# Attention and two MoE blocks on one core: q and k given head dimension first, scores from stacked high and low parts

## What is computed

```python
scores = scale * np.matmul(q, k.transpose(0, 1, 3, 2))      # scale = 1/8
rel = pos[:, None] - pos[None, :]
bias = slopes[:, None, None] * (-np.abs(rel).astype(np.float32))[None, :, :]
mask = (rel >= 0) & (rel < 128)
scores = np.where(mask, scores + bias[None], -1000000000.0)
attn = exp(scores - max) / (sum + 1e-09)
x = (attn @ v) as (2304 tokens, 512)
x = relu(x @ w_in) ** 2 @ w_out                             # w_in 512 x 2048
logits = x @ w_gate ... P from 8 rounds of row and column sums
out += P[:, e:e + 1] * (relu(x @ w1[e]) @ w2[e])            # 8 experts, 1024 wide
```

## Time and profile before

| what | value |
|---|---|
| three runs | 2126.38, 2123.18, 2125.97 us, median 2125.97 |
| profiled execution | 2127.54 us, its span 2125.8 us |
| TensorE busy | 98% of the span, weight loads 89% |
| VectorE, ScalarE, POOL busy | 62%, 39%, 58% |
| granted TensorE clock, mean | 0.995 |

### The profile page before, as it was taken

One profiled execution on the slowest core, in us unless ns is written; L12 is line 12 of the kernel. 1 busy time (PEld: TensorE's weight loads), 2 busy tenths in 40 slices (PEclk: granted clock), 3 DMA queues, 4 the chain that ended last, 5 costly groups with the idle time before them and its releaser, 6 DMA issues.

```text
span 2125.8 us, 37567 instructions
## 1 busy us (share of the span) xinstructions
PE 2085.9 (98%) x11906; PEld 1881.9 (89%) x11906; DVE 1310.8 (62%) x2729; ACT 821.1 (39%) x1643; POOL 1227.6 (58%) x1604
## 2 busy tenths in 40 slices
PE   7899999999999999999999999999999999999999
PEld 3799898899998998999988999899998999989898
DVE  7566665676657655565665655556566565655655
ACT  5565565564532332333332323333333333323332
POOL 3122322224457666666776666666676766676663
PEclk9999999999999999999999999999999999999999
DMA  5232332322222122222222222222222222222221
GB/s 125 67 83 61 99 85 78 88 78 60 85 65 60 61 69 69 69 69 69 67 63 98 65 64 69 69 69 69 68 66 94 70 69 66 64 67 69 69 69 60
DMA packets 208145, 154.55 MB, mean 73 GB/s; under 512 B 66464, under 2 KB 164768, under 8 KB 208032
## 3 DMA queue, kind: packets, MB, share of 16 engines
q1 hardware_dynamic: 208032, 153.15, 24.7%
HBM read 148.39 MB, written 4.72 MB: 72 GB/s over the span
## 4 chain that ended last, share of the span: by engine, by line
PE 92%; DVE 3%; issue 2%; ACT 1%; POOL 1%; DMA 0%; SPq 0%; DVEq 0%; ACTq 0%; POOLq 0%
PE bank L788 36%; PE bank L749 32%; PE bank L688 10%; PE bank L681 9%; PE bank L646 2%; PE bank L672 1%; PE bank L657 1%; DVE relu L1156 1%; ACT prob L884 1%; DVE prob L1089 0%; PE bank L617 0%; DVE prob L1119 0%; POOL el L564 0%; DVE g1l L1131 0%; DVE gl L1232 0%
## 5 line engine op out<-in xcount | busy, mean ns | idle before, releaser
L564 POOL TENSOR_TENSOR el<-ew,eh 128x256 fp32r<-128x256 f32 x672 | 471.8, 738 | 293.5 <-ACT eh L852 293.5
L1275 DVE SCALAR_TENSOR_TENSOR z_sb<-bank,gate,z_sb 128x512 f32<-128x512 f32 x540 | 403.7, 749 | 248.1 <-PE bank L788 248.1
L749 PE MATMUL bank<-xh,eh 128*128 128x384 f32 x1344 | 451.0, 336 | 3.5 <-DVE gl L1232 3.5
L749 PE MATMUL bank<-xh,el 128*128 128x384 f32 x1344 | 450.8, 335 | 0.0
L788 PE MATMUL bank<-fh,gh 128*128 128x512 f32 x1152 | 450.4, 391 | 0.4 <-DVE z_sb L1275 0.4
L788 PE MATMUL bank<-fh,gl 128*128 128x512 f32 x1152 | 450.7, 391 | 0.0
L788 PE MATMUL bank<-fl,gh 128*128 128x512 f32 x1152 | 450.5, 391 | 0.0
L749 PE MATMUL bank<-xl,eh 128*128 128x384 f32 x1344 | 450.3, 335 | 0.0
L502 POOL TENSOR_TENSOR wl<-stage,wh 128x512 fp32r<-128x512 f32 x120 | 159.8, 1332 | 372.8 <-ACT wh L852 372.8
L574 POOL TENSOR_TENSOR fl<-fw,fh 128x256 fp32r<-128x256 f32 x384 | 274.4, 746 | 133.6 <-ACT fh L852 133.3
L852 ACT ACTIVATE p<-bank 128x384 f32<-128x384 f32 x96 | 47.2, 492 | 654.0 <-PE bank L749 654.0
(11 more groups left out here) (130 smaller groups left out, 2985.4 us busy)
## 6 DMA issues: line engine op xcount, KB each, us to landing
fw<-in_moe_w_dram SPq DMA_DIRECT2D x96, 512.0 KB, 3.6
ew<-in_moe_w_dram SPq DMA_DIRECT2D x96, 256.0 KB, 2.8
stage<-in_moe_w_in_dram SPq DMA_DIRECT2D x64, 256.0 KB, 3.0
stage<-in_moe_w_out_dram SPq DMA_DIRECT2D x64, 256.0 KB, 2.8
a<-in_moe_w_dram SPq DMA_DIRECT2D x96, 128.0 KB, 2.7
ew<-in_moe_w_dram SPq DMA_DIRECT2D x96, 128.0 KB, 2.9
k_raw<-in_k_dram SPq DMA_DIRECT2D x32, 128.0 KB, 2.7
q_raw<-in_q_dram SPq DMA_DIRECT2D x32, 128.0 KB, 2.5
```

What stands on the lines that cost most here:

```text
L564: last = pool.tensor_tensor(el[r][:, a, :, :], ew[r][:, a, :, :], f(eh[r][:, a, :, :]), ALU.subtract)
L749: done = pe.matmul(ps, w[r][:, a, kc, :], x[:, b, kc, :], start=(first and kc == 0 and w is eh and x is xh), stop=(kc == 1 and w is el), s ...
L1275: dve.scalar_tensor_tensor(out=z, in0=ps, scalar=weight, in1=z, op0=ALU.mult, op1=ALU.add).then_inc(z_free, 1)
```

## The change

numpy hands q and k over as (batch, heads, head dimension, positions), so the head dimension can go onto partitions without a transpose. For batch 0 all four pairs are loaded at once into `qT0` and `kT0`, two heads on 2 x 64 partitions, and the scores of each head are one fp32 product over its 64 partitions, into two banks. For the other batches each head's 64 rows are loaded twice, onto both halves of the partitions. The k tiles become the high part in both halves (`k_hh`) and the low part in both (`k_ll`); the q tile has the high part in one half and the low part in the other (`q_hl`). A product over 128 partitions of `q_hl` with `k_hh` is high plus low of q by high of k, and with `k_ll` by low of k. So a head takes two products of 256 columns, where three products of 512 columns served two heads. Rounds are two now, k then q, with no TensorE part. The scale of 1/8 moves into the bias tiles and the bias addition; six of the eight bias tiles move to POOL, and the distances get a tile of their own. SP's list puts the first batch's loads ahead.

```diff
-    ROUNDS = 3
+    ROUNDS = 2
...
+        qT0 = sb("qT0", [P, KC, QT * P], fp32, W0 + 2 * WS)
+        kT0 = sb("kT0", [P, KC, QT * P], fp32, placed["qT0"])
+        dist = sb("dist", [P, 2 * P], fp32, placed["kT0"])
...
+        q_twice = sb("q_twice", [P, 2, S], fp32, placed["bias"])
+        k_twice = sb("k_twice", [P, 2, S], fp32, placed["q_twice"])
+        q_hl = sb("q_hl", [P, 2, QT * P], fp32r, placed["k_twice"])
+        k_hh = sb("k_hh", [P, 2, QT * P], fp32r, placed["q_hl"])
+        k_ll = sb("k_ll", [P, 2, QT * P], fp32r, placed["k_hh"])
...
+        s_ps, s_odd, pT_ps = [bank[0], bank[4]], [bank[6], bank[7]], [bank[1], bank[5]]
...
                 ev.append(("slot", j))
-                c, r = j // QT + 1, j % QT - 1
-                if c < KC and 0 <= r < ROUNDS:
-                    ev.append(("round", c, r))
...
-            apart = (0, 2, 5)
+            apart = (0, 2)
...
+            def load_first(c):
+
+                for tile, src in ((kT0, kf), (qT0, qf)):
+                    sp.dma_start(tile[:, c, 0:S], src[2 * c:2 * c + 2, :, :].rearrange("h d s -> (h d) s")
+                                 ).then_inc(first_in[c], 16)
+
+            def load_twice(pair, raw, src, there):
+
+                for half in range(2):
+                    sp.dma_start(raw[half * D:(half + 1) * D, :, :],
+                                 src[bass.ds(pair * 2, 2), :, :].rearrange("h d s -> d h s")).then_inc(there, 16)
...
 
-                        wait_alone(sp, t_done, b * (KC * ROUNDS) + (a[0] + 1) * ROUNDS)
-                        load(b * KC + (a[0] + 1), k_raw, kf, k_in)
-                        load(b * KC + (a[0] + 1), q_raw, qf, q_in)
+                        wait_alone(sp, qk_lo, b * (KC * ROUNDS) + (a[0] + 1) * ROUNDS)
+                        load_twice(b * KC + (a[0] + 1), k_twice, kf, k_in)
+                        load_twice(b * KC + (a[0] + 1), q_twice, qf, q_in)
...
-            load(0, k_raw, kf, k_in)
-            load(0, q_raw, qf, q_in)
+            load_first(0)
             sp.wait_ge(v_zero, 1)
+            load_v(0, 0)
+            load_first(1)
+            load_v(1, 1)
+            load_first(2)
+            load_first(3)
...
+            pool.wait_ge(dist_ready, 1)
+            pool.wait_ge(bias_ready, 2)
+            for h in range(2, H):
+                pool.tensor_scalar(bias[:, h, :], dist[:, :], float(2.0 ** (-8.0 * (h + 1) / H)) / SCALE, MASKED / SCALE,
+                                   ALU.mult, ALU.max).then_inc(bias_ready, 1)
+            for z in (q_hl, k_hh, k_ll):
+                pool.memset(f(z[:, :, S:]), 0.0).then_inc(zeros_later, 1)
...
+            pe.wait_ge(zeros_ready, 2)
...
-                s, (nq, k0) = c % n, span(t)
-                if t == 0:
-                    pe.wait_ge(t_lo, b * (ROUNDS * KC) + ROUNDS * c + 2)
-                if t == FULL:
-                    pe.wait_ge(t_lo, b * (ROUNDS * KC) + ROUNDS * (c + 1))
+                _, k0 = span(t)
+                if plain(b) and t == 0:
+                    pe.wait_ge(first_in[c], 32)
+                if not plain(b) and t == 0:
+                    pe.wait_ge(qk_lo, b * (ROUNDS * KC) + ROUNDS * (c + 1))
                 bank_wait(neg_done, b, j, n)
-                o = s_ps[j % n][:, :].rearrange("p (h k) -> p h k", h=2)[:, :, k0:]
-                n0 = (t - 1) * P + k0
-                if plain(b):
-                    products = ((qT0[:, s, :], kz0[:, s, :, :]),)
-                else:
-                    products = ((qTh, kzh), (qTh, kzl), (qTl, kzh))
-                for i, (x, y) in enumerate(products):
-                    last = pe.matmul(o, x[:, t * P:(t + 1) * P], y[:, :, n0:(t + 1) * P],
-                                     start=(i == 0), stop=(i == len(products) - 1))
+                at, keys = slice(t * P, (t + 1) * P), slice((t - 1) * P + k0, (t + 1) * P)
+                for h in range(2):
+                    d = slice(h * D, (h + 1) * D)
+                    if plain(b):
+                        last = pe.matmul((s_ps, s_odd)[h][j % n][:, k0:2 * P], qT0[d, c, at], kT0[d, c, keys],
+                                         start=True, stop=True)
+                        continue
+                    for y in (k_hh, k_ll):
+                        last = pe.matmul(s_ps[j % n][:, h * 2 * P + k0:(h + 1) * 2 * P], q_hl[:, h, at], y[:, h, keys],
+                                         start=(y is k_hh), stop=(y is k_ll))
                 last.then_inc(s_done, 1)
...
-                    if what == "round":
-                        transpose_round(b, *a)
...
+            def round_hi(b, c, r):
+
+                if r == 0:
+                    act.wait_ge(s_done, b * STEPS + c * QT)
+                act.wait_ge((k_in, q_in)[r], (b - 1) * (32 * KC) + 32 * (c + 1))
+                tile, raw = ((k_hh, k_twice), (q_hl, q_twice))[r]
+                copy(tile[:, :, 0:S], raw[:, :, :]).then_inc(qk_hi, 1)
...
+            for tile in (qT0, kT0):
+                dve.memset(tile[:, :, S:], 0.0).then_inc(zeros_ready, 1)
...
+            for h in range(2):
+                dve.tensor_scalar(bias[:, h, :], dist[:, :], float(2.0 ** (-8.0 * (h + 1) / H)) / SCALE, MASKED / SCALE,
                                   ALU.mult, ALU.max).then_inc(bias_ready, 1)
-            dve.wait_ge(bias_ready, H)
+            dve.sem_inc(qk_lo, ROUNDS * KC)
             dve.sem_inc(y_free, 2)
...
+            def round_lo(b, c, r):
+
+                dve.wait_ge(qk_hi, (b - 1) * (ROUNDS * KC) + (ROUNDS * c + r + 1))
+                tile, high, raw, d = ((k_ll, k_hh, k_twice, slice(0, P)), (q_hl, q_hl, q_twice, slice(D, P)))[r]
+                dve.tensor_tensor(tile[d, :, 0:S], raw[d, :, :], f(high[d, :, 0:S]), ALU.subtract).then_inc(qk_lo, 1)
...
+                if plain(b) and h == 0 and j % QT == 0:
+                    dve.wait_ge(bias_ready, 2 * (j // QT) + 2)
+                scored = (s_ps, s_odd)[h][j % n][0:nq, k0:2 * P] if plain(b) else \
+                    s_ps[j % n][0:nq, h * 2 * P + k0:(h + 1) * 2 * P]
                 last = dve.tensor_tensor_reduce(
-                    out=prob[0:nq, j % 2, h, k0:], in0=s_ps[j % n][0:nq, h * 2 * P + k0:(h + 1) * 2 * P],
-                    in1=bias[0:nq, 2 * (j // QT) + h, k0:], scale=-1.0, scalar=3.0e38,
+                    out=prob[0:nq, j % 2, h, k0:], in0=scored,
```

More of the change, by code:

```diff
@@ L194, in attention_moe_moe_kernel @@
         pool_chain = sem("pool_chain")
+        first_in = [sem(f"first_in{c}") for c in range(KC)]
         q_in = sem("q_in")
@@ L197, in attention_moe_moe_kernel @@
         v_in = [sem(f"v_in{r}") for r in range(2)]
[L198 to L200 removed]
+        qk_hi = sem("qk_hi")
+        qk_lo = sem("qk_lo")
         s_done = sem("s_done")
@@ L295, in alone_events @@
         def alone_events():
-            ev = [("v", 0), ("v", 1)] + [("round", 0, r) for r in range(ROUNDS)]
+            ev = [("v", 0), ("v", 1)]
             for j in range(SLOTS):
                 ev.append(("slot", j))
-                c, r = j // QT + 1, j % QT - 1
-                if c < KC and 0 <= r < ROUNDS:
-                    ev.append(("round", c, r))
                 ev += v_after(j)
@@ L360, in _, with load_v @@
         def _(sp):
[L361 to L368 removed]
+            def load_first(c):
[6 more added lines that the diff above has]
+                                 src[bass.ds(pair * 2, 2), :, :].rearrange("h d s -> d h s")).then_inc(there, 16)
+            def load_v(pair, c):
+                for h in range(2):
+                    one = vf[bass.ds(pair * 2 + h, 1), :, :].rearrange("o s d -> (o s) d")
+                    sp.dma_start(v_sb[:, c % 2, 0:FULL, h * D:(h + 1) * D],
+                                 one[0:FULL * P, :].rearrange("(t p) d -> p t d", p=P)).then_inc(v_in[c % 2], 16)
+                sp.dma_start(v_sb[0:TAIL, c % 2, FULL, :].rearrange("p (h d) -> p h d", h=2),
+                             vf[bass.ds(pair * 2, 2), FULL * P:S, :].rearrange("h p d -> p h d")
+                             ).then_inc(v_in[c % 2], 16)
             def load_piece(src, n, r):
@@ L605, in _ @@
             pe.wait_ge(ident_ready, 1)
-            pe.wait_ge(zeros_ready, 3)
-            def transpose_round(b, c, r):
-                if r < 2:
-                    pe.wait_ge((k_in, q_in)[r], b * (3 * 16 * KC) + 3 * 16 * (c + 1))
-                if not isinstance(b, int) or c or r:
-                    wait_alone(pe, t_lo, b * (ROUNDS * KC) + (ROUNDS * c + r))
-                if r < 2:
-                    raw = (k_raw, q_raw)[r]
-                    for t in range(FULL):
-                        last = pe.transpose(t_ps[:, t * P:(t + 1) * P],
-                                            raw[:, t, :, :].rearrange("p h d -> p (h d)"), ident[:, :])
-                else:
-                    for i, raw in enumerate((q_raw, k_raw)):
-                        last = pe.transpose(t_ps[:, i * TAIL:(i + 1) * TAIL],
```

(17 more changed lines are left out.)

106 lines of the change are left out of this document (20 added, 86 removed).

## The result

The changed kernel takes 2132.24 us (median of 20 runs), the kernel before 2126.12 (20 runs): ratio 1.0032, 95% interval [1.0024, 1.0039]. It is slower by 0.3%, where 2108 was forecast, with a range of 2095 to 2119 and a chance of 0.05 for slower. Its profiled span is 2130.0 us.

A forecast was written before the change was run, and what follows sets the result against it. TensorE was taken to bound the windows and the softmax loop the alone stretch. 7.5 us won there plus 10.2 in the windows made 17.7, from a median of 2125.97 to 2108, range 2095 to 2119 (8 in 10).

The forecast's parts named there:

- What bounds it: TensorE makes 92% of the chain; softmax loop paces the alone stretch; in the windows fewer streamed columns save time.
- Start of the alone stretch: Batch 0's attention alone: without transposes the first bias addition comes at 6.6 us, 5.5 won (4.5 to 6.4).
- Its slots: Alone stretch, slots after the first bias addition: 5.8 us excess, 2 of it won with the rounds (0 to 5.8).
- rival B: Alone stretch wins nothing: with less work TensorE's clock falls to 1.2 GHz and stays; 9 won, 2117; chance 0.12.
- Scores, copies, low parts: Windows: score products 0.12 apart, copies of 1.15, low parts of 1.34, wait for q's low part near 1, six times.
- Rival C: Windows: low parts held by POOL subtractions, 1.66 more a hold, 15 in all; slower than before, 2133; chance 0.05.
- Pair 0: First pair of a window: both big transposes and the old stall (1.67) bring only 0.1; y bank free no sooner.
- Hidden, 0: Windows: doubled k and q loads, issued four or five slots early, cost 0; without cover a pair waits 2.5 us or longer.
- The sum: Whole kernel: alone stretch 7.5 plus windows 10.2 makes 17.7 won, 2108 for the median; chance 0.62.

The follow-up runs named there:

- x1_turn: Changed kernel with the q and k loads at a window's head held back until TensorE finished the window's first layer-1 group: 2130.91 us.
- x2_spaced: Changed kernel with the next pair's loads taken apart, k's four groups behind the k round's place and q's eight behind: 2125.90 us.
- z1_after_pad: Changed kernel with only 32 already met waits ahead of TensorE's first product, so the loop head stands 16 instructions later: 2123.49 us.
- x3_both: Changed kernel with the edits of x1_turn and x2_spaced together: 2121.58 us.
- x6_pad: x3_both with 32 already met waits ahead of TensorE's first product, so the loop head stands 16 instructions later: 2115.50 us.
- x11_piece_late: x6_pad with the weight piece behind groups 18 and 42 moved behind the round that follows group 19 and 43: 2112.17 us.
- x12_best: x8_all with 32 met waits replacing its idle products, and window weight pieces behind each unit's third layer-1 group moved behind the fourth: 2109.81 us.
- x8_all: x3_both with rounds and slots of pairs 0 to 2 moved, and 8 idle TensorE products ahead of the first scores: 2111.82 us.
- x9_all_fill: x8_all with one more idle product behind the scores of every slot of the alone stretch: 2111.57 us.
- y2_before_pad: Kernel before with 490 already met waits ahead of TensorE's first instruction, putting the loop head at the changed kernel's place in a block: 2155.22 us.

## Why the prediction was wrong

**What bounds it** was read rightly: time went wherever TensorE waited, and its own work fell by 15.8 us in the windows.

**Start of the alone stretch: right, and just above its bounds.** 4.5 to 6.4 us were expected, 6.7 came. The loads landed by 4.48, inside the 4.3 to 6.2, but from the scores to the bias addition it took 0.99, where 1.42 was kept from before. The first bias addition is at 5.47, from 12.17 in the earlier trace rows:

```profile
4.48 2.88 PE L646 MATMUL bank<-kT,qT 64*128 64x128 f32 x12 [4.48 <-DMA qT<-in_q_dram]
...
5.47 0.29 DVE L1054 CUSTOM_DVE_ANT_0 prob<-bank,bias 128x128 f32<-128x128 f32 x1 [1.67 <-PE bank L646]
```

**Its slots: wrong, by rival B's mechanism.** "I give 2 of the 5.8 to the rounds" failed by 4.6 us: 4.1 were won by the end of the stretch. TensorE ran at half clock until 44.8 us, where the kernel before did so until 14.4 and from 21.2 to 24.7. The 0.94 that the page gives for both stretches hides this: the trace's clock records begin at 44.8 and at 14.4 us, each with 1.00, and what lies ahead of the first record counts as 1.00. The durations show it. The kernel before, then the changed one:

```profile
19.93 0.63 PE L657 MATMUL bank<-ident,prob 128*128 128x128 f32 x4 [1.76 <-DVE prob L1119]
```

```profile
42.33 1.09 PE L661 MATMUL bank<-ident,prob 128*128 128x128 f32 x4
45.16 0.63 PE L661 MATMUL bank<-ident,prob 128*128 128x128 f32 x4
```

From the transposes at 10.87 to those at 42.33 us ten slots took 3.15 us each; from 45.16 to 47.51 it was 2.35. The same code of this stretch ended between 60.45 and 66.01 us in ten profiles (3.6 to 9.1 won), and that goes with the first clock record: 44.8 to 48.4 us in the changed kernel, x1_turn, x2_spaced and z1_after_pad, which end at 65.4 to 66.0, and 15.0 to 30.9 in the other six, which end at 60.5 to 63.8. This is a correlation; no run was made to set the clock's rise alone. Why it rises so much later in some runs was not found, so part of any of these medians can be this stretch and not the edit.

**Scores, copies, low parts: right.** Score products follow in 0.12 (104.29, 104.41), copies take 1.15 to 1.17, low parts 1.36 at the median, and the wait for q's low part is 0.88 at six places. Rival C's form, the low parts of q and k held by POOL, hardly came: three of 24 took 1.59.

**Pair 0: right.** Of its 1.67 only 0.1 should stay, because the y bank comes free no sooner. There are now waits of 0.34 for `g1l` and 1.07 for the y bank instead of 0.85 and 0.82 of transposes. From the window's first product to its ninth group, that is over pair 0's two rounds, the first window takes 16.20 us (65.43 to 81.63) after 16.26 (69.57 to 85.83).

**"Hidden, 0", the loads: wrong.** Issued "four or five slots early" they are hidden for q and k, but the weight piece behind them in SP's queue is not, and behind its late copy stand relu, square and `g1l`. I had costed the loads at their user, and wrote that the weight loads behind them would come earlier; the one behind pair 1's loads came later. x2_spaced measured 4.7 us of windows, and the loads at the turn another 3.8 (x3_both).

**Left out altogether: the loop's head.** This is the largest step that failed: no term stood for it, which put it at nothing. Eleven instructions fewer ahead of the loop put its head just before a block's end: 6.3 us of windows by x6_pad against x3_both, 11.0 by z1_after_pad, where the loads at the turn lengthen the second fetch. The two turns stood in the trace of before as one gap each, and removed instructions were counted as a gain only.

**The g1l waits: right mechanism, wrong instruction.** Rival C's hold was priced on the low parts; it struck the `g1l` two instructions behind k's, and TensorE waited 0.8 to 1.1 for it, six times. The price of 1.66 was too high for this place: the instance of 2.117 stands at 523.27 us, in the last window, beside POOL subtractions of 1.84 on `acc`, while `g1l` takes 1.53, 1.08 more, beside the weight subtraction. The long instances of the earlier trace rows were there to be asked which of their neighbours would now run late.

**The sum.** The windows were to win 10.2 and lost 11.5, 21.7 apart. x2_spaced, x3_both and x6_pad take 14.8 of it away (555.7 to 540.9). Of the 6.9 left x11_piece_late takes 3.9. The last 3.0, and more, lie at the turn: from the start of the last four second-layer groups ahead of a turn to the start of the first four behind it, x6_pad takes 4.8 us more than the kernel before over both turns and x11_piece_late 5.2, with a longer single gap and a half-clock spell behind it that the kernel before has not. The rest of the windows wins 12.4 in x11_piece_late where 10.2 was forecast (1.0 of it in the last window, where nothing was changed). In the changed kernel itself the two turns, measured like this, lose 12.5 us, the second-layer groups at the three late pieces lose 6.6, and all other groups together win 7.5. With all mended, x12_best stands at 2109.8, close to the 2108 of the forecast; but as a forecast of this kernel it was wrong.

## What to carry to other kernels

When a change adds or removes instructions ahead of a long hardware loop, look at where the loop's head falls against the fetch blocks before judging the change: here 16 instructions that do nothing were worth 8.7 us, more than the whole of what the change was measured to lose. Price a load by what is queued behind it, not by its own user alone. And when a long VectorE step is moved in, ask for each SBUF-to-SBUF step behind it which POOL instruction it will now meet.

## What was not expected of the hardware

- A turn of a loop of some 2,330 TensorE instructions shows one gap of 1.5 to 3.7 us without a wait, or two (2.56 + 4.00 in the changed kernel) when its head stands 12 instructions ahead of a block's end. Data loads of 1180 KB issued at the same time lengthen the second by 1.6 to 1.9 us (x1_turn). A single gap they did not lengthen: it is 2.00 and 2.51 with them in z1_after_pad, 2.43 and 3.62 without them in x6_pad.
- The granted clock of the page says nothing ahead of the trace's first clock record. From 10 to 20 us of the changed kernel, whose first record is at 44.8, it reads 1.00 (2.4 GHz), beside these rows:

```profile
13.69 1.09 PE L661 MATMUL bank<-ident,prob 128*128 128x128 f32 x4
14.71 1.12 PE L676 MATMUL bank<-pT,v_sb 128*64 128x128 f32 x8
```

  where the kernel before takes 0.63 and 0.66 for the same shapes at 37 us. In x8_all and x9_all_fill, whose records begin at 6.9 and 5.8, the reading of 0.50 (1.2 GHz) and the 1.09 go together. At the start of a trace durations of equal shapes are the surer guide.
- 490 met waits, 245 instructions, put TensorE's first product at 28.43 us instead of 4.34, 0.1 us for each instruction (y2_before_pad).
